# A retention layer and two expert layers in one kernel: the last tile's hidden values turned in the middle of the output products of the tile in front of it

## The reference, cut to what matters

```python
# 1 retention over B=4, H=8, S=576, 64 per head
ret = (q @ k.T / sqrt(64)) * Dmat          # decay by distance, causal
x = (ret @ v) laid out as 2304 rows of 512
# 2 dense layer, 512 -> 2048 -> 512
h = x @ w_in
x = (max(h, 0) + log1p(exp(-abs(h)))) @ w_out
# 3 eight experts, two for each row, 512 -> 1024 -> 512
noisy = x @ w_gate + log1p(exp(x @ w_noise)) * noise
top2, weights = the two largest of noisy, softmax over the two
for e in range(8):
    out[rows of e] += weight * (relu(x[rows of e] @ w1[e]) @ w2[e])
```

## Time and profile before

| | us |
|---|---|
| median of three runs | 1023.05 |
| the profiled execution's own time | 1022.97 |
| its span in the profile | 1021.1 |
| TensorE busy | 1005.7 |
| VectorE, ScalarE, GpSimd busy | 396.3, 430.6, 208.3 |
| mean granted clock of TensorE | 0.998 |

### The profile page before, as it was taken

The page is one execution under the profiler, slowest core; times in us unless marked ns, Lnnn a source line. Parts: engine busy times, 40 slices in busy tenths (PEclk is TensorE's granted clock), DMA queues, the critical chain, the costliest instruction groups (busy, mean ns, idle before and its releaser), DMA issues.

```text
span 1021.1 us, 22022 instructions
## 1 busy us (share of the span) xinstructions
PE 1005.7 (98%) x5982; PEld 871.4 (85%) x5983; DVE 396.3 (39%) x784; ACT 430.6 (42%) x736; POOL 208.3 (20%) x198
## 2 busy tenths in 40 slices
PE   9999999999999999999999999999998999999996
PEld 7889999999999999999888888888887888888885
DVE  3565632432532423425553222242366354222221
ACT  3337754544555455557532222242354453222221
POOL 4540000020010200200332222222322232322222
PEclk9999999999999999999999999999999999999999
DMA  8753450000000000052316222243277342211111
GB/s 272 253 170 125 147 190 1 1 32 0 0 31 0 0 31 0 10 207 90 117 33 223 68 62 64 66 137 132 88 243 256 121 156 73 82 52 52 52 48 45
DMA packets 47078, 95.27 MB, mean 93 GB/s; under 512 B 19245, under 2 KB 24749, under 8 KB 42928
## 3 DMA queue, kind: packets, MB, share of 16 engines
q1 hardware_dynamic: 24240, 66.26, 19.2%
q0 software_dynamic: 10992, 27.84, 8.6%
q10 hardware_dynamic: 11808, 0.68, 0.8%
HBM read 78.98 MB, written 20.37 MB: 97 GB/s over the span
## 4 chain that ended last, share of the span: by engine, by line
PE 92%; DMA 3%; issue 2%; POOL 1%; ACTq 1%; DVE 0%; ACT 0%; SPq 0%; DVEq 0%; POOLq 0%
PE bank L701 27%; PE bank L703 26%; PE bank L702 26%; PE bank L833 3%; PE bank L780 2%; PE bank L652 2%; PE bank L626 2%; PE bank L756 1%; DMA xg<-x_rows,meta_x 1%; PE bank L645 1%; PE bank L612 1%; PE bank L665 1%; DMA out<-ysb,meta_y 1%; PE bank L750 1%; DMA lists<-rec,slot 0%
## 5 line engine op out<-in xcount | busy, mean ns | idle before, releaser
L701 PE MATMUL bank<-ew,hT_hi 128*128 (+1 forms) x328 | 131.9, 402 | 2.6 <-DVE hT_lo L1432 2.6
L701 PE MATMUL bank<-ew,xgT_hi 128*128 (+1 forms) x328 | 131.9, 402 | 0.7 <-issue 0.7
L701 PE MATMUL bank<-xs_hi,mw 128*128 (+1 forms) x384 | 130.0, 338 | 0.0
L703 PE MATMUL bank<-xs_hi,mw 128*128 (+1 forms) x384 | 129.6, 337 | 0.0
L702 PE MATMUL bank<-xs_lo,mw 128*128 (+1 forms) x384 | 129.0, 336 | 0.0
L703 PE MATMUL bank<-ew,xgT_lo 128*128 (+1 forms) x328 | 128.5, 392 | 0.0
L703 PE MATMUL bank<-ew,hT_lo 128*128 (+1 forms) x328 | 128.4, 391 | 0.0
L702 PE MATMUL bank<-ew,hT_hi 128*128 (+1 forms) x328 | 127.8, 390 | 0.0
L702 PE MATMUL bank<-ew,xgT_hi 128*128 (+1 forms) x328 | 127.6, 389 | 0.0
L520 POOL DMA_INDIRECT lists<-rec,slot x36 | 35.8, 994 | 389.5 <-DVE slot L1336 380.3
L701 PE MATMUL bank<-mw,g_hi 128*128 128x512 f32 x288 | 115.1, 399 | 0.0
(11 more groups left out here) (185 smaller groups left out, 1664.1 us busy)
## 6 DMA issues: line engine op xcount, KB each, us to landing
raw<-w_ex SPq DMA_DIRECT2D x32, 1024.0 KB
stage<-w_ff SPq DMA_DIRECT2D x16, 512.0 KB, 3.4
out<-blank SPq DMA_DIRECT2D x3, 1536.0 KB, 11.4
x_rows<-x2sb SPq DMA_DIRECT2D x6, 768.0 KB, 3.9
kbuf<-kN SPq DMA_DIRECT2D x16, 256.0 KB, 3.2
vbuf<-vN SPq DMA_DIRECT2D x16, 256.0 KB, 4.7
qbuf<-qT SPq DMA_DIRECT2D x15, 256.0 KB, 3.9
xg<-x_rows,meta_x POOLq DMA_INDIRECT x43
```

Of the source, the lines that this page charges most:

```text
L701: pe.matmul(o, a_hi, b_hi, start=first, stop=False)
L703: return pe.matmul(o, a_lo, b_hi, start=False, stop=last)
```

## The change

The hidden values of the last tile of an odd count are no longer turned after the output products of the tile in front, but in the middle of them.

- `expert_out` can be told to stop after 12 of its 24 matmuls, run `hidden_transpose` of another tile, and go on with the other 12 (`between`).
- The table has a new row `T_PRIOR`, (tiles - 3) >> 1, which is one less than `T_PAIR`; VectorE makes it with two more small operations. TensorE's and VectorE's loops run to it, one pass fewer than before, and the last pass is written out. ScalarE, GpSimd and SyncE keep their loops.
- After its loop TensorE reads six entries (three tiles), makes step 0 of the written-out pass, reads three entries, and makes step 1 with the new `expert_out`.
- The high and low halves of tile 2 * pair go to `hE_hi` and `hE_lo0`, which lie in a place of their own, and `hE_lo1`, which lies over the first tile's turned rows. So ScalarE's copies for it no longer wait for the output products in front. On VectorE its low halves are made ahead of `add_output` of the tile in front.
- Where there is one more tile, it uses `hT_hi` and `hT_lo` in place of `hE_hi` and `hE_lo`.

Left out of the diff below: three places where ScalarE's calls name the count that they wait for, which is the count of before.

```diff
--- before.py
+++ after.py
@@ -165,9 +165,11 @@
         prev, a = place("prev", [P, 2, D], F32, a)
         ysb, a = place("ysb", [P, 2, D], F32, a)
         assert a <= R_C
-        hE_hi, hE_at = place("hE_hi", [P, FT2, P], F32R, R_T + 2 * D * 4)
-        hE_lo, hE_at = place("hE_lo", [P, FT2, P], F32R, hE_at)
-        assert hE_at <= R_T + 2 * D * 4 + 4 * KT * P * 4
+        hE_hi, a = place("hE_hi", [P, FT2, P], F32R, a)
+        hE_lo0, a = place("hE_lo0", [P, FT2 // 2, P], F32R, a)
+        hE_lo1, hE_end = place("hE_lo1", [P, FT2 // 2, P], F32R, R_T + 2 * D * 4)
+        assert a <= R_C and hE_end <= R_T + 2 * D * 4 + KT * P * 4
+        hE_lo = (hE_lo0, hE_lo1)
 
         square, a = place("square", [P, 3, P], F32, R_C)
         ident, earlier, allrows = square[:, 0, :], square[:, 1, :], square[:, 2, :]
@@ -221,7 +223,7 @@
         t_gx, a = place("t_gx", [LANES, ROUNDS, E], F32, a)
         t_v, a = place("t_v", [LANES, 12, ROUNDS], F32, a)
         assert a <= R_W
-        T_E, T_ROW, T_PAR, T_PAIR, T_TWO = range(5)
+        T_E, T_ROW, T_PAR, T_PAIR, T_TWO, T_PRIOR = range(6)
         T_FIRST, T_NEXT, T_SPLIT, T_LOAD = 0, 1, (2, 3), (4, 5)
         L_FIRST, L_SECOND, L_ROW = 0, 1, 2
         GATE_STEPS, GAP_STEP = 16, 4
@@ -833,18 +835,26 @@
                     last = pe.transpose(hT_ps[k // 4][:, k % 4, :], hid[:, k * P:(k + 1) * P], ident)
                 last.then_inc(hT_made, 1)
 
-            def expert_out(g, e, par, h_hi=hT_hi, h_lo=hT_lo):
-                pe.wait_ge(w_lo_done[1], e * 2 + 2)
-                at_least(pe, y_done, g)
-                for k in range(FT2):
+            def expert_out_part(g, e, par, ks, h_hi, h_lo):
+                for k in ks:
                     if k % 4 == 0:
                         pe.wait_ge(hT_lo_done, g * 2 + k // 4 + 1)
                     cols = bass.ds(KT * F2 + k * D, D)
-                    last = three(y_ps, h_hi[:, k, :], h_lo[:, k, :],
+                    last = three(y_ps, h_hi(k), h_lo(k),
                                  ew[:, bass.ds(par, 1), 0, cols].rearrange("p o n -> p (o n)"),
                                  ew[:, bass.ds(par, 1), 1, cols].rearrange("p o n -> p (o n)"),
                                  k == 0, k == FT2 - 1)
-                last.then_inc(m2_done, 1)
+                return last
+
+            def expert_out(g, e, par, h_hi=lambda k: hT_hi[:, k, :], h_lo=lambda k: hT_lo[:, k, :], between=None):
+                pe.wait_ge(w_lo_done[1], e * 2 + 2)
+                at_least(pe, y_done, g)
+                if between is None:
+                    expert_out_part(g, e, par, range(FT2), h_hi, h_lo).then_inc(m2_done, 1)
+                else:
+                    expert_out_part(g, e, par, range(FT2 // 2), h_hi, h_lo)
+                    hidden_transpose(between)
+                    expert_out_part(g, e, par, range(FT2 // 2, FT2), h_hi, h_lo).then_inc(m2_done, 1)
 
             def step(i, s, this, after):
                 g = 2 * i + s
@@ -897,21 +907,27 @@
             tile_transpose(3, 1, 2)
             step(1, 0, early[0], early[1])
             step(1, 1, early[1], early[2])
-            with pe.Fori(2, pair) as i:
+            prior = entry(pe, T_PRIOR, 0, PAIR_LOW - 1, PAIR_HIGH - 1)
+            with pe.Fori(2, prior) as i:
                 first, second = slot_of(2 * i), slot_of(2 * i + 1)
                 step(i, 0, first, second)
                 third = slot_of(2 * i + 2)
                 step(i, 1, second, third)
 
-            first, second = slot_of(2 * pair), slot_of(2 * pair + 1)
+            first, second, third = (slot_of(2 * prior + k) for k in range(3))
+            step(prior, 0, first, second)
             two = entry(pe, T_TWO, 0, 0, 1)
-            hidden_transpose(2 * pair)
+            fourth = slot_of(2 * prior + 3)
+            hidden_transpose(2 * prior + 1)
+            expert_in(2 * prior + 2, 0, *third)
+            tile_transpose(2 * prior + 3, 1, prior + 2)
+            expert_out(2 * prior + 1, *second, between=2 * prior + 2)
             with pe.If(two):
-                expert_in(2 * pair + 1, 1, *second)
-                hidden_transpose(2 * pair + 1)
-            expert_out(2 * pair, *first)
+                expert_in(2 * prior + 3, 1, *fourth)
+                hidden_transpose(2 * prior + 3)
+            expert_out(2 * prior + 2, *third, lambda k: hE_hi[:, k, :], lambda k: hE_lo[k // 4][:, k % 4, :])
             with pe.If(two):
-                expert_out(2 * pair + 1, *second, hE_hi, hE_lo)
+                expert_out(2 * prior + 3, *fourth)
 
 
         @block.scalar
@@ -1066,12 +1082,11 @@
                 nc.scalar.activation(hid[:, 0:512], m1_ps[0], ACT.Relu)
                 nc.scalar.activation(hid[:, 512:1024], m1_ps[1], ACT.Relu).then_inc(relu_done, 1)
 
-            def split_hidden(g, end=False):
-
-                h_hi = hE_hi if end else hT_hi
+            def split_hidden(g, done=0, h_hi=hT_hi):
+
                 act.wait_ge(hT_made, g + 1)
-                if not end:
-                    at_least(act, m2_done, g)
+                if done is not None:
+                    at_least(act, m2_done, done)
                 for k in range(2):
                     nc.scalar.activation(h_hi[:, 4 * k:4 * k + 4, :], hT_ps[k], ACT.Copy).then_inc(hT_hi_done, 1)
 
@@ -1100,7 +1115,7 @@
             def step(i, s):
 
                 g = 2 * i + s
-                split_hidden(g)
+                split_hidden(g, g)
                 split_weights(g + 1, 0)
                 split_tile(g + 2, s)
 
...
@@ -1165,11 +1180,11 @@
                 for s in range(2):
                     step(i, s)
 
-            split_hidden(2 * pair)
+            split_hidden(2 * pair, None, hE_hi)
             with act.If(entry(act, T_TWO, 0, 0, 1)):
                 split_weights(2 * pair + 1, 0)
                 next_tile(pair, 0)
-                split_hidden(2 * pair + 1, True)
+                split_hidden(2 * pair + 1, 2 * pair)
             alone(act, ld_mx[1], pair * 16 + 32)
 
 
@@ -1426,11 +1441,11 @@
             split_tile(1, 1)
             keep_x2(NCH - 1)
 
-            def split_hidden(g, h_hi=hT_hi, h_lo=hT_lo):
+            def split_hidden(g, h_hi=hT_hi, h_lo=(hT_lo[:, 0:4, :], hT_lo[:, 4:8, :])):
                 for k in range(2):
                     dve.wait_ge(hT_hi_done, 2 * g + k + 1)
-                    dve.tensor_tensor(h_lo[:, 4 * k:4 * k + 4, :], hT_ps[k],
-                                      as32(h_hi[:, 4 * k:4 * k + 4, :]), ALU.subtract).then_inc(hT_lo_done, 1)
+                    dve.tensor_tensor(h_lo[k], hT_ps[k], as32(h_hi[:, 4 * k:4 * k + 4, :]), ALU.subtract
+                                      ).then_inc(hT_lo_done, 1)
 
             def add_output(i, s, rows_there=True):
 
@@ -1501,9 +1516,12 @@
                                      ALU.mult, ALU.add)
             tabled(dve.tensor_tensor_scan(t_end[:, :], t_one[:, :], t_seq[:, :], 0.0, ALU.mult, ALU.add))
             dve.tensor_scalar(t_last[:, 0:1], t_end[:, E - 1:E], -1.0, None, ALU.add)
+            dve.tensor_scalar(t_last[:, 1:2], t_end[:, E - 1:E], -3.0, None, ALU.add)
             tabled(dve.tensor_tensor(t_ge[:, :, 0:E - 1], spread(tile_no, 2, shape),
                                      spread(t_end[:, 0:E - 1], 1, shape), ALU.is_ge))
             dve.tensor_scalar(col(cols, T_PAIR), t_last[:, 0:1].broadcast_to([LANES, ROUNDS]), 1, None,
+                              ALU.arith_shift_right)
+            dve.tensor_scalar(col(cols, T_PRIOR), t_last[:, 1:2].broadcast_to([LANES, ROUNDS]), 1, None,
                               ALU.arith_shift_right)
             dve.tensor_scalar(col(cols, T_TWO), t_last[:, 0:1].broadcast_to([LANES, ROUNDS]), 1, None,
                               ALU.bitwise_and)
@@ -1563,30 +1581,32 @@
                         dve.tensor_tensor(part(1), raw[:, w], as32(part(0)), ALU.subtract
                                           ).then_inc(w_lo_done[p], 1)
 
-            def step(i, s):
+            def step(i, s, end=False):
                 g = 2 * i + s
                 split_hidden(g)
                 split_weights(g + 1, 0)
                 split_tile(g + 2, s)
                 split_weights(g, 1)
+                if end:
+                    split_hidden(g + 1, hE_hi, [t[:, :, :] for t in hE_lo])
                 add_output(i, s)
 
             dve.wait_ge(tab_done, 1)
             dve.wait_ge(tab2_done, 1)
-            pair = entry(dve, T_PAIR, 0, PAIR_LOW, PAIR_HIGH)
-            with dve.Fori(1, pair) as i:
+            prior = entry(dve, T_PRIOR, 0, PAIR_LOW - 1, PAIR_HIGH - 1)
+            with dve.Fori(1, prior) as i:
                 for s in range(2):
                     step(i, s)
-
-            two = entry(dve, T_TWO, 0, 0, 1)
-            split_hidden(2 * pair)
-            with dve.If(two):
-                split_weights(2 * pair + 1, 0)
-                split_weights(2 * pair, 1)
-                split_hidden(2 * pair + 1, hE_hi, hE_lo)
```

(17 more changed lines are left out.)

## The result

| | before | after |
|---|---|---|
| median | 1023.95 us (20 runs) | 1027.39 us (20 runs) |
| profiled span | 1021.1 us | 1025.1 us |

The ratio is 1.0033 with a 95% interval of 1.0025 to 1.0042: 3.4 us slower, 2.6 to 4.3. I had forecast 1024.7 us, 1.7 us slower than before, with a range up to 1025.7. The sign was right, the amount was half of what came, and the time lies outside the range. Of the 2.7 us between 1024.7 and 1027.39, 0.9 us are the kernel before itself: its median was 1023.05 in the three runs that I started from and 1023.95 in these twenty. Against that, the change is still 1.8 us slower than forecast, and 0.8 us slower than the range allowed.

The account below looks back on a forecast made before the run. The prediction took the chain from tile 39's last product through add, scatter, gather and tile 40's add to bound the end; 0.93 + 0.75 = 1.68 us on the profiled 1022.97, plus 0.08 for the median, gave 1024.7 us, range 1023.4 to 1025.7.

Parts of the forecast that it names:

- What bounds the end: Kernel's end: the chain leaves TensorE at tile 39's last product, then add, scatter, gather and add of tile 40.
- The closed part of the hole: TensorE's 1.52 us idle before tile 40's output products: off the last chain, so nothing it gives back arrives.
- Term 1: Tile 40's eight transposes amid tile 39's products: they delay those products' end by 0.93 us, bounds 0.79 to 1.03.
- The relu: Tile 40's relu, needed by its transposes: ends 0.30 us before the twelfth product gives way; no wait taken.
- Term 2: TensorE's loop end: a sixth table read makes tile 38's transposes 0.75 us late, bounds 0 to 0.9.
- rival 1: TensorE's loop end: the sixth read is hidden because the sequencer runs further ahead or catches up; 1024.0 us, chance 0.16.
- The cover on VectorE: VectorE before tile 39's add: done with tile 40's low halves 0.35 us before its add; called thin.
- Rival 3: VectorE: tile 39's add waits behind tile 40's low halves; 1025.7 us for half, 1026.6 for all; chance 0.10.
- Sum: Chain to the kernel's end: 0.93 + 0.75 = 1.68 us added, nothing off, giving 1024.7 us.

Follow-up runs that it names:

- e2: Changed kernel with four table entries instead of six read between the loop and tile 38's transposes, the others later; ratio to the kernel before 1.0025.
- e1: Changed kernel plus 77 TensorE instructions ahead of its last loop, all but five jumped over, so its code page comes sooner; ratio to the kernel before 1.0027.
- e3: Changed kernel with tile 40's transposes behind all 24 products of tile 39 again, VectorE's changed order kept; ratio to the kernel before 1.0056.
- e10: Odd-count version making tile 40's hidden values by halves around tile 39's output products, four reads after the loop, no padding; ratio to the kernel before 0.9980.
- e7: Changed kernel with four reads after the loop, 78 jumped-over instructions, transposes behind tile 39's products, VectorE's add before the low halves; ratio to the kernel before 1.0000.

## Why the prediction was wrong

Point by point:

- What bounds the end: right. The chain still leaves TensorE at the end of tile 39's products, tile 40's add waits for the gather (9.5 us in the trace of after), and TensorE is done 3.4 us before it; almost 2 were foretold, and the slow scatter gives the rest. The closed part of the hole gave nothing.
- Term 1, 0.93 us: right, 0.86 measured. The relu was in time.
- Term 2, 0.75 us for the sixth read: right, 0.79 measured from start to start (0.64 of them idle, a little under the 0.7 to 0.9 foretold), and e2 takes it away. So rival 1, a longer lead, didn't hold here: the loop's branch is taken at 978.4, 4.7 us ahead of the transposes at 983.14, and less their 0.8 us of lateness that is the lead of 4.0 us seen before.
- The cover on VectorE: 0.35 us foretold, 0.33 us of idle time before the add in e1 and after alike. Rival 3 didn't happen, and e3 shows what it is like.
- **The step that failed is in "Sum": the scatter's time.** I took the chain behind tile 39's add as it stood ("as long from there"), and bounded the scatter by 2.3 to 2.8 us, its landings from 900 us on in a trace in which no page of code fell on one. It took 4.51 us. The change makes TensorE's program longer, and so moves its pages; one was fetched at 1011.97 in the kernel before too, behind the scatter, where the gather took 3.30 us, little more than the 3.1 to 3.3 of the other traces. The prediction doesn't weigh the fetch of code at all, in any term or rival. TensorE lost nothing by it; it took a DMA engine from the scatter. That is 1.74 us in this trace, 0.8 to 1.7 in the four traces in which it happened. That a scatter on this chain can be slow stood in the trace of before too: outside the stretch that I looked at, the one issued at 702.25 took 4.7 us, beside a load of weights issued at 700.87 (DMA share 0.72, against 0.24 around the scatter at 909.81, which took 2.77).
- The starting point: 0.9 us of the miss are the median of the kernel before, as said above. That is no step of the mechanism.

## What to carry to other kernels

An edit that adds instructions to an engine can move the later fetches of its code; on TensorE each was a 16 KB packet here, and those near tile 39's scatter took 1.0 to 1.6 us on one DMA engine. Where a transfer spread over all 16 engines is on the critical path, look for the instruction queues in the DMA view of that stretch, before and after, and for an unexplained loss try a block that is jumped over ahead of it. And before closing a hole on a busy engine, see which moment on that engine the last chain leaves from: work put in front of it costs in full, and work taken from in front of it is what pays (2.2 us in the trace of e10).

## What the runs showed of the hardware

- Tile 39's scatter of 128 rows by 2 KB landed in 2.76 to 2.78 us in eight of the nine traces in which no page of q8 met its data (3.15 in e7, unexplained), and in 3.54, 4.04, 4.10 and 4.51 us with a page starting 2.8 to 3.1 us behind the add. It had landed 1.35 to 1.52 us behind the page's end. With the page at +1.4 and at +4.2 us there was no loss.
- Each table entry read by TensorE's sequencer takes 0.75 us, and the sequencer ran some 4 us ahead of the matmuls. Between the loop and the transposes four reads cost nothing (e2), five just so (before), and the sixth was paid in full (0.79 us, after).
- In e3, behind 2.96 us without a matmul, the granted clock was 0.56 and 0.72 in the next two stretches (about 3 us of products at 1.2 GHz) and 1.00 again from 1016 us. Behind the idle times of 1.5 us in the kernel before and 1.1 us in the changed one it was 1.00.
